# Other rounds for the weight splits of the first expert, for the scatters of two batches and for one weight load, in a fused attention and mixture-of-experts kernel

## What is computed

```python
scores = scale * np.matmul(q, k.transpose(0, 1, 3, 2))
scores = np.where(is_sink | in_window, scores, -1000000000.0)
a = np.exp(scores - np.max(scores, axis=-1, keepdims=True))
a = a / (np.sum(a, axis=-1, keepdims=True) + 1e-09)
x = np.matmul(a, v)                       # (3072 tokens, 512)
expert_idx = np.argmax(x @ w_gate, axis=1)
for e in range(8):
    h = np.maximum(x[mask] @ w1[e], 0.0)
    out[mask] = gate_w[mask, None] * (h @ w2[e])
h = out @ w_in
return (h - np.tanh(h)) @ w_out
```

## Time and profile before

| | us |
|---|---|
| median of 3 runs | 1077.38 |
| the runs | 1075.28 to 1077.5 |
| the profiled execution | 1071.83 |
| its span, first to last instruction | 1070.1 |
| attention stage of the span, rounds 0 to 23 and their end | about 0 to 175 |

### The profile page before, as it was taken

The page is one execution under the profiler, slowest core; times in us unless marked ns, Lnnn a source line. Parts: engine busy times, 40 slices in busy tenths (PEclk is TensorE's granted clock), DMA queues, the critical chain, the costliest instruction groups (busy, mean ns, idle before and its releaser), DMA issues.

```text
span 1070.1 us, 17027 instructions
## 1 busy us (share of the span) xinstructions
PE 1058.0 (99%) x5919; PEld 866.1 (81%) x5919; DVE 651.6 (61%) x1393; ACT 474.8 (44%) x1013; POOL 504.2 (47%) x522
## 2 busy tenths in 40 slices
PE   9999999999999999999999999999999999999997
PEld 6777777888888888888888888888888888888885
DVE  7898895343343434443498666766666666676664
ACT  7988885242143333441644333333333333333332
POOL 4575674661070725770654453444335335344532
PEclk9999999999999999999999999999999999999999
DMA  9647634543142516462411110100101011000001
GB/s 309 205 140 249 215 129 144 197 132 125 51 168 90 197 56 213 169 221 64 140 50 60 51 40 0 42 17 23 30 11 40 11 31 40 1 1 21 20 1 40
DMA packets 38491, 100.16 MB, mean 94 GB/s; under 512 B 8464, under 2 KB 9104, under 8 KB 33296
## 3 DMA queue, kind: packets, MB, share of 16 engines
q1 hardware_dynamic: 29680, 52.68, 15.7%
q0 software_dynamic: 8448, 46.27, 12.2%
q10 hardware_dynamic: 288, 0.26, 0.1%
HBM read 76.06 MB, written 23.13 MB: 93 GB/s over the span
## 4 chain that ended last, share of the span: by engine, by line
PE 91%; DVE 5%; issue 2%; DMA 1%; POOL 1%; ACT 0%; POOLq 0%; DVEq 0%
PE bank L875 24%; PE bank L883 24%; PE bank L818 14%; PE bank L804 14%; PE bank L527 3%; PE bank L565 2%; PE bank L810 2%; PE bank L542 2%; DVE prob L1188 2%; PE bank L791 1%; DVE probT L1204 1%; DMA sorted_x<-x_tok,dest 1%; PE bank L859 1%; PE bank L687 1%; PE bank L589 0%
## 5 line engine op out<-in xcount | busy, mean ns | idle before, releaser
L1673 POOL TENSOR_TENSOR weights<-raw,weights 128x1024 fp32r<-128x1024 f32 x70 | 166.6, 2399 | 187.3 <-ACT weights L943 178.0
L883 PE MATMUL bank<-weights,gT_hi 128*128 128x512 f32 x768 | 238.7, 392 | 0.2 <-DVE gT_lo L1539 0.2
L1796 POOL TENSOR_SCALAR ser<-ser 128x512 f32<-128x512 f32 x96 | 61.6, 642 | 281.0 <-DVE ser L1484 280.9
L875 PE MATMUL bank<-mT_hi,weights 128*128 128x512 f32 x768 | 189.8, 389 | 0.7 <-ACT mT_hi L1112 0.7
L875 PEld LDWEIGHTS bank<-mT_hi,weights 128*128 128x128 f32 x768 | 144.1, 188 | 30.8 <-ACT mT_hi L1112 0.9
L883 PEld LDWEIGHTS bank<-weights,gT_hi 128*128 128x128 f32 x768 | 142.6, 188 | 29.4 <-DVE gT_lo L1539 0.7
L883 PE MATMUL bank<-weights,gT_lo 128*128 128x512 f32 x384 | 149.7, 390 | 0.0
L1126 ACT ACTIVATE bank<-bank 128x512 f32<-128x512 f32 x96 | 55.9, 582 | 210.1 <-DVE ser L1515 210.1
L818 PE MATMUL bank<-weights,hT_hi 128*128 128x512 f32 x448 | 143.5, 401 | 0.0
L804 PE MATMUL bank<-weights,mT_hi 128*128 128x512 f32 x448 | 140.8, 395 | 0.0
L1798 POOL TENSOR_SCALAR sq<-sq 128x512 f32<-128x512 f32 x94 | 140.5, 1495 | 0.0
(11 more groups left out here) (188 smaller groups left out, 1581.8 us busy)
## 6 DMA issues: line engine op xcount, KB each, us to landing
raw<-w_all POOLq DMA_DIRECT2D x32, 1024.0 KB, 5.4
raw<-w_all SPq DMA_DIRECT2D x8, 1024.0 KB, 7.2
sorted_y<-ys SPq DMA_DIRECT2D x30, 261.0 KB, 3.1
xs<-sorted_x SPq DMA_DIRECT2D x29, 261.0 KB, 2.8
v_in<-vt SPq DMA_DIRECT2D x24, 256.0 KB, 3.7
kT<-kt SPq DMA_DIRECT2D x23, 264.0 KB, 3.8
qT<-qt SPq DMA_DIRECT2D x23, 256.0 KB, 4.5
raw<-sorted_y SPq DMA_DIRECT2D x20, 261.0 KB, 2.6
```

Of the source, the lines that this page charges most:

```text
L875: done = e.matmul(bank[HB[n % 3]][:, :], wt[:, f // 2, c, cols], x[:, c, :], start=(m == 0), stop=(m == 3 * CH - 1))
L883: done = e.matmul(bank[YB[i]][:, :], x[:, n % 3, rows], wt[:, f, :], start=(f == 0 and m == 0), stop=(f == GCH - 1 and m == 2))
L1673: e.tensor_tensor(lo, src, hi.bitcast(F32), ALU.subtract).then_inc(s_w_lo, 1)
L1796: e.tensor_scalar(row, row, SERIES_2, 1.0, ALU.mult, ALU.add).then_inc(s_ser, 1)
```

## The change

Three tables of numbers change, and the loop that reads one of them so that a round may hold two low splits. The number of instructions of each kind stays the same.

```diff
-    HI_IN, LO_IN, RAW_AT = (4, 5, 6, 6, 12, 12, 18, 18), (5, 6, 8, 9, 14, 15, 20, 21), (16, 17, 18, 23)
+
+    HI_IN, LO_IN, RAW_AT = (4, 5, 6, 8, 9, 10, 11, 12), (5, 6, 11, 11, 12, 12, 17, 18), (16, 17, 18, 20)
...
-
                         n = i - LAST[b] - 5
-                        first = (0, 1, 2, 6) if b < 2 else (0, 3, 6, 6)
+                        first = (0, 2, 4, 6) if b < 2 else (0, 3, 6, 6)
...
-                if i in LO_IN:
-                    split_lo(0, LO_IN.index(i))
+                for y, at in enumerate(LO_IN):
+                    if at == i:
+                        split_lo(0, y)
```

## The result

The changed kernel takes **1079.27 us** (median of 12 runs, 1075.94 to 1084.43); the kernel before, in runs beside it, 1075.76 us (12 runs, 1074.01 to 1077.50). The ratio is 1.0033, 95% interval 1.0021 to 1.0044: slower by 3.5 us, a third of a per cent, and more than can be mistaken for no change.

A forecast was written before the change was run, and what follows sets the result against it. TensorE, busy 99% at full clock, was taken to bound the kernel. Terms of +2.7, -0.40 and -0.65 us gave +1.65, added to a median of 1077.38 for 1079.0 us; range 1076.2 to 1081.2.

The forecast's parts named there:

- Within 0.2%: Whole kernel: the time differs from the kernel before by no more than 2.15 us; chance 0.61.
- slower: Whole kernel: slower than the kernel before by more than 2.15 us; chance 0.30.
- the clock falling behind the gap: Round 14, sign of being wrong: TensorE's clock drops after its idle gap of about 2 us.
- the wait of L1212: Round 13, expected sign: VectorE waits once, about 4 us, for GpSimd's cast of the sink values.
- Part 1: Rounds 11 and 12, two low splits each: GpSimd's later cast delays VectorE, less one scatter wait; +2.7 us.
- by 94.5: Round 14: the last scatter of batch 0 lands by then, before VectorE's inversion asks for it.
- TensorE's clock falls: Rival, round 14: the idle gap drops the clock to 1.2 GHz, costing some 3 us, at most 7; chance 0.08.
- Part 2: Rounds 17 and 18, one split each, scatters two by two: VectorE's scatter wait in round 20 goes; -0.40 us.
- Part 3: Rounds the low splits leave: merges collide less with VectorE's casts L1280 and L1294; together -0.65 us.
- three times 0.31: Rounds 9, 15 and 21: bound on the gain from shorter L1294 casts, -0.9 us; -0.3 was taken.
- Part 4: High splits on ScalarE moved to rounds 8 to 11: nothing, up to +0.5 us if a merge comes late.
- Part 5: Raw load moved to round 20, ahead of tile 21's keys and queries: nothing, up to +1 us if late.

The follow-up runs named there:

- kernel 1: The changed kernel run again without any edit: 1074.31 us against 1071.02 for the kernel before, ratio 1.0031.
- kernel 2: The kernel before, unaltered and profiled anew: 1070.77 us against 1070.89, ratio 0.9998.
- kernel 9: The kernel before with only the scatters of batches 0 and 1 issued two by two: 1070.62 us against 1071.02, ratio 1.0000.
- kernel 10: The changed kernel with low splits and raw loads as in the kernel before, leaving new scatters and high splits: 1069.74 us against 1070.89, ratio 0.9988.
- kernel 7: The changed kernel with round 12's two low splits put back to rounds 14 and 15: 1071.36 us against 1070.89, ratio 1.0004.
- 4, cast, one split: As kernel 3, but one of the two low splits of round 12 moved to round 14: 1070.87 us against 1070.89, ratio 1.0001.
- kernel 5: The changed kernel with nine extra unread matmuls in TensorE's gap in round 14: 1073.07 us, ratio 1.0022 to the kernel before.
- 6, changed, four matmuls: The changed kernel with four extra unread matmuls in round 14 instead of nine: 1077.60 us against 1075.59 for the kernel before, ratio 1.0026.
- kernel 3: The changed kernel with GpSimd's cast of the sink values issued ahead of the low splits: 1073.90 us, ratio 1.0022 to the kernel before.
- 8, only the pair of round 12: The changed kernel with round 11's two low splits put back to rounds 8 and 9: 1074.10 us against 1075.59 for the kernel before, ratio 0.9994.
- 11, all but Part 1: The changed kernel with low splits of rounds 11 and 12 back in 8, 9, 14, 15: 1075.23 us against 1075.59, ratio 0.9998.
- 12, and raw load as before: The changed kernel with low splits back in rounds 8, 9, 14, 15 and the raw load in round 23: 1075.47 us against 1075.59, ratio 0.9998.

## Why the prediction was right and wrong

The time, 1079.0, is 0.3 us from the measured 1079.27, and that is luck: two errors of opposite sign. The prediction stood on a median of 1077.38 from three runs, 5.55 us above the profile, and with 12 runs it is 1075.76, 3.93 above; that is 1.6 us too much. What was predicted was a difference of +1.65 us, and it is +3.5 (+3.3 in kernel 1); that is 1.9 us too little. "Within 0.2%" had 0.61 and did not come true; "slower" had 0.30, and 0.22 of that for other reasons than the one that came. The text had named the clock falling behind the gap as a sign of being wrong, and it fell. The other signs came as said: the wait of L1212, the gap, no wait for scatters, the cast at 0.17 us, and no wait of TensorE for keys or queries of tile 21.

The steps of TensorE from one tile's values to the next tell where. Differences from kernel 2, in us:

| kernel | to tile 13 | to tile 14 | to tile 19 | to tile 21 | tile 12 to 23 | time |
|---|---|---|---|---|---|---|
| 9, scatters alone | -0.12 | -0.39 | -0.01 | -0.01 | -0.56 | -0.40 |
| 10, and high splits | -0.34 | -0.39 | -0.30 | +0.01 | -1.06 | -1.15 |
| 7, pair of round 11 | +0.85 | -0.01 | -0.30 | -0.22 | +0.30 | +0.47 |
| 4, cast, one split | +0.39 | 0.00 | -0.30 | -0.21 | -0.13 | -0.02 |
| 5, changed, clock held | +2.54 | -0.39 | -0.30 | -0.21 | +1.59 | +2.05 |
| 6, changed, four matmuls | +2.48 | -0.38 | -0.30 | -0.22 | +1.53 | +2.01 |
| 3, changed, cast first | +2.99 | +0.37 | -0.30 | -0.22 | +2.79 | +2.88 |
| 1, changed | +3.12 | +0.52 | -0.30 | -0.22 | +3.07 | +3.29 |
| 8, only the pair of round 12 | -0.35 | -0.39 | -0.29 | -0.22 | -1.30 | -1.49 |
| 11, all but Part 1 | -0.35 | -0.38 | -0.29 | -0.22 | -1.17 | -0.36 |
| 12, and raw load as before | -0.35 | -0.39 | -0.30 | -0.22 | -1.18 | -0.12 |

The last column is the difference of the medians from the kernel before on the same chip; it follows the column before it within 0.5 us, but for the kernels 11 and 12.

- **The sum without the clock came out, by errors that cancelled.** With the clock held, kernel 5 is +1.59 us (+2.05 by the times) where +1.65 was worked out. Part 1's mechanism and place stand, and its size nearly: the queue through the rounds 11 and 12 ends at 95.27, where its items added up to 95.31 and 95.5 was taken. In the two steps to tile 13 and 14 kernel 5 is +2.54 - 0.39 = +2.15; if the high splits' 0.22 (below) is in that, Part 1 alone is +2.37 against the +2.7 taken and the 2.55 that was to be its least. The inversion, from which 2.7 was worked out, is 2.48 us later in the changed kernel (96.37 against 93.89). The scatters land later than "by 94.5" (kernel 7 waits for them until 95.17), but still before VectorE asks.
- **The step that failed is the clock.** The rival "TensorE's clock falls" had 0.08. It came true in every profile with a gap of 2 us, and costs 1.5 us by the traces (kernel 1 less kernel 5: 0.58 and 0.91 in the two steps) and 1.24 by the times, which is not clear of their noise; "some 3 us, at most 7" was too much. The term was put at nothing in the sum, and with the measured 1.5 us it would have been +3.1, against +3.3 to +3.5 measured. The text itself had the gap (2.1 to 2.7 us) and the fact that no trace of before holds a gap over 1.1 us. An effect that nothing before could show is not made unlikely by that. The Trainium skill (TensorE: Matmul & The Clock Gate, "What's actually happening") had said that an idle TensorE goes back to half rate, and the trace agrees with 0.57; 0.08 was too little for it.
- **Part 2, -0.40, was nothing**: the wait of round 20 is in one of the two profiles of the kernel before and in no other kernel. Part 1's credit for the scatter wait of round 14 (0.57) was real (0.46 in kernel 2, and gone in kernel 9).
- **Part 3, -0.65, was -0.2**, at tile 21, where the low splits leave the rounds 20 and 21. The cast at the end of round 21 took 0.17 us, as said, and 0.66 in all four profiles that have splits in these rounds (both of the kernel before, kernels 9 and 10). But L1295 in the same round took 0.54 us in the changed kernel, longer than any of the earlier trace rows. In round 15 it took 0.17 where it had been 0.48, a gain as forecast, and TensorE's step there moved by 0.05 us at most: a shorter cast is not always a shorter round. The bound "three times 0.31" took every case for the longest; the casts of the rounds 9, 15 and 21 were 0.33, 0.48 and 0.47.
- **Part 4, nothing, was -0.50**: 0.22 at tile 13 and 0.30 at tile 19, where ScalarE loses pairs of splits. I looked for the harm in the rounds that receive splits and not for the relief in those that lose them.
- **Part 5, nothing, was nothing** (kernels 11 and 12). But the 5.55 us of the median over the profile, taken as untouched by the change, were no fixed amount: 3.93 with 12 runs of the kernel before, and 1.54 for the changed kernel, whose profile has the late stall.

So the errors of the Parts 1 to 4 cancelled one another (+2.37, 0, -0.2 and -0.5 in place of +2.7, -0.40, -0.65 and 0), and the one term that was left out of the sum, the clock, made the miss in the difference.

No kernel here beats the kernel before by more than 0.2%; the best by its ratio, kernel 10, is 0.12% faster, and the only faster one whose interval does not reach 1.

## What to carry to other kernels

When a moved instruction opens a gap on TensorE, price two things: the gap, and the clock behind it. Here 2.1 us of gap cost some 1.5 us more, 1.2 us of gap left the clock alone, and a few matmuls that nobody reads gave the difference back, by the traces. A long GpSimd instruction delays a VectorE instruction with two SBUF inputs both from in front (its result is awaited) and from the side (kernel 3), so changing their order alone cures nothing; the queue must be shorter at that point (kernels 4 and 8). A wait that is seen in one profile only should not be booked as a gain before a second profile has shown it. And a time that comes out right says little when the difference behind it does not.

## What was not expected of the hardware

- VectorE's L1212, 0.68 us alone, lasted 4.36 us beside two GpSimd splits and 2.06 us beside one. It waited through the change from one split to the next.
- The granted clock fell to 0.86 and 0.57 after TensorE had been idle for 2.08 us, and not after 1.22 us. It was lower behind each of the eight gaps of 1.99 us or more.
- On one of the three chips of the experiments every profile has a stall of 2.4 us at the end of the attention stage, with no event that released it, and the clock behind it falls to 0.50 to 0.75 in the lowest stretch of 5 us; the kernel before was 4.6 us slower there.
